# Writing the zero rows in eight pieces in steps 4 to 6, with batch 0's scatter moved to step 7

## What is computed

```python
p_packed = sm_attn(p, k, v)              # 8 batches, 8 heads: 32 packs attend to 576 tokens
out      = sm_attn(q, p_packed, p_packed)  # 576 tokens attend to the 32 packed values
x = out.transpose(0, 2, 1, 3).reshape(4608, 512)
# mixture of experts, the best one of 8 for each token
expert = argmax(x @ w_gate, axis=1)
x[expert == e] = gate * (relu(x[expert == e] @ w1[e]) @ w2[e])
# dense part on all tokens
r = relu(x @ w_in)                       # 512 -> 2048
y = (s * r * r + b) @ w_out              # 2048 -> 512
```

## Time and profile before

| | us |
|---|---|
| Median of three runs | 1540.14 |
| Lowest and highest | 1539.99 and 1545.33 |
| The profiled execution | 1553.64 |
| Its span, first to last instruction | 1551.9 |
| PE busy in the span | 1458.8 |
| Attention, to the last scatter issued | 197 |
| First slot's rows landed | 203.5 |

### The profile page before, as it was taken

One profiled execution on the slowest core, in us unless ns is written; L12 is line 12 of the kernel. 1 busy time (PEld: TensorE's weight loads), 2 busy tenths in 40 slices (PEclk: granted clock), 3 DMA queues, 4 the chain that ended last, 5 costly groups with the idle time before them and its releaser, 6 DMA issues.

```text
span 1551.9 us, 24717 instructions
## 1 busy us (share of the span) xinstructions
PE 1458.8 (94%) x8664; PEld 1174.5 (76%) x8665; DVE 474.2 (31%) x808; ACT 480.3 (31%) x973; POOL 415.6 (27%) x278
## 2 busy tenths in 40 slices
PE   6887369999999999998999999999999999999996
PEld 5655258888888888886888888888888888888885
DVE  3777621111111111113523232322323232332322
ACT  5666123333333333332222222222222222222221
POOL 0244678448266557104501010100101010010100
PEclk9899679999999999999999999999999999999998
DMA  9688345234243343212101010100101000000000
GB/s 309 220 264 250 120 147 159 87 108 133 70 141 108 109 122 115 81 48 90 61 14 42 7 41 14 38 10 14 41 8 41 14 34 14 14 27 0 27 1 27
DMA packets 52860, 122.93 MB, mean 79 GB/s; under 512 B 6609, under 2 KB 12753, under 8 KB 52817
## 3 DMA queue, kind: packets, MB, share of 16 engines
q1 hardware_dynamic: 33728, 79.21, 16.8%
q10 hardware_dynamic: 13136, 24.19, 5.1%
q0 software_dynamic: 5952, 18.92, 3.4%
HBM read 90.78 MB, written 31.52 MB: 79 GB/s over the span
## 4 chain that ended last, share of the span: by engine, by line
PE 90%; DVE 3%; issue 3%; DMA 1%; POOL 1%; ACT 1%; another core or an unknown queue 0%; SPq 0%; ACTq 0%; DVEq 0%; POOLq 0%
PE psum L674 18%; PE psum L676 18%; PE psum L675 18%; PE psum L750 8%; PE psum L748 8%; PE psum L749 8%; PE psum L718 2%; PE psum L507 1%; PE psum L683 1%; PE psum L736 1%; PE psum L568 1%; PE psum L547 1%; POOL x_by_expert L418 1%; PE psum L609 1%; PE psum L622 1%
## 5 line engine op out<-in xcount | busy, mean ns | idle before, releaser
L1241 DVE SCALAR_TENSOR_TENSOR s_r_r<-r_relu,s_col 128x512 f32<-128x512 f32 x144 | 116.1, 806 | 450.4 <-ACT r_relu L972 450.4
L482 POOL DMA_INDIRECT out_dram<-out_sb,out_row_of_y x36 | 36.0, 1001 | 747.2 <-ACT out_sb L982 739.0
L674 PE MATMUL psum<-weights_split,gT_hi 128*128 128x512 f32 x576 | 230.8, 401 | 2.3 <-DVE gT_lo L1243 2.2
L972 ACT ACTIVATE r_relu<-psum 128x512 f32<-128x512 f32 x144 | 86.1, 598 | 471.7 <-PE psum L750 456.9
L675 PE MATMUL psum<-weights_split,gT_hi 128*128 128x512 f32 x576 | 227.7, 395 | 0.0
L676 PE MATMUL psum<-weights_split,gT_lo 128*128 128x512 f32 x576 | 227.6, 395 | 0.0
L750 PE MATMUL psum<-yT_hi,weights_split 128*128 128x512 f32 x576 | 227.2, 394 | 0.0
L748 PE MATMUL psum<-yT_hi,weights_split 128*128 128x512 f32 x576 | 226.1, 393 | 0.1
L749 PE MATMUL psum<-yT_lo,weights_split 128*128 128x512 f32 x576 | 225.8, 392 | 0.0
L396 POOL TENSOR_TENSOR weights_split<-weights_raw,one 128x1024 fp32r<-128x1024 f32 x70 | 135.5, 1936 | 253.9 <-PE psum L676 242.7
L398 POOL TENSOR_TENSOR weights_split<-weights_raw,weights_split 128x1024 fp32r<-128x1024 f32 x70 | 170.0, 2428 | 5.5
(11 more groups left out here) (151 smaller groups left out, 1832.4 us busy)
## 6 DMA issues: line engine op xcount, KB each, us to landing
weights_raw<-in_moe_w_dram SPq DMA_DIRECT2D x64, 512.0 KB
x_slot<-x_by_expert ACTq DMA_DIRECT2D x40, 257.0 KB, 2.8
y_sorted<-y_slot ACTq DMA_DIRECT2D x40, 256.5 KB, 3.3
k_sb<-in_k_dram SPq DMA_DIRECT2D x16, 576.0 KB, 6.5
q_sb<-in_q_dram SPq DMA_DIRECT2D x16, 576.0 KB, 7.7
v_sb<-in_v_dram SPq DMA_DIRECT2D x48, 192.0 KB
y_tile<-y_sorted SPq DMA_DIRECT2D x32, 256.5 KB, 2.7
weights_raw<-in_moe_w_in_dram SPq DMA_DIRECT2D x8, 512.0 KB
```

Source lines behind the costliest of these rows:

```text
L674: nc.tensor.matmul(dst, lhs[0][:, col:col + P], rhs[0], start=first_, stop=False)
L972: nc.scalar.activation(rel[:], ps[:, HFB + par, :], ACT.Relu).then_inc(rel_done, 1)
L1241: nc.vector.scalar_tensor_tensor(sq[par][:], rel[:], s_col[:], rel[:], ALU.mult, ALU.mult).then_inc(sq_done, 1)
```

## The change

The single DMA of zeros ahead of step 0 is gone. ACT issues eight DMAs of 128 rows (257 KB) in its place: three in step 4, three in step 5, two in step 6, each group after `out_q` (and `exp_logits`) and before `out_pkt`. Each raises `zeroed` by 16, and POOL waits for 128. POOL no longer issues batch 0's scatters between the work of batches 1 and 2. It does `round_low(2)` after the sum of batch 1's logits, then the sum of batch 2's logits, the wait on `zeroed`, and all six scatters of batch 0 in a row, followed by batch 1's as before.

```diff
             for b in range(1, B):
                 u = 2 * b + 2
-                if b >= 2:
+                if b >= 3:
                     if b + 1 < B:
                         pool.wait_ge(pk_done, u + 1)
                     scatter(b - 2, 4)
...
                 sum_logits(b)
                 if b == 1:
-                    pool.wait_ge(zeroed, 16)
-                if b + 1 < B:
+                    round_low(2)
+                if b == 2:
+                    pool.wait_ge(zeroed, 16 * E)
+                    for j in range(J):
+                        scatter(0, j)
+                if 2 <= b and b + 1 < B:
                     scatter(b - 1, 0)
                     pool.wait_ge(m1_done, min(u + 3, UNITS))
                     scatter(b - 1, 1)
...
             out_kq(0)
-            act.wait_ge(zeros_done, 1)
-            act.dma_start(rows_dram.rearrange("(e r) c -> r e c", e=E)[0:P],
-                          zeros[:].unsqueeze(1).to_broadcast([P, E, XW])).then_inc(zeroed, 16)
             for it in range(UNITS + 1):
                 if it < UNITS:
                     out_q(it)
                 if it >= 5 and it % 2 == 1:
                     exp_logits((it - 5) // 2)
+                if it == 4:
+                    act.wait_ge(zeros_done, 1)
+                if 4 <= it < 7:
+                    for e in range(3 * it - 12, min(3 * it - 9, E)):
+                        act.dma_start(rows_dram[e * REG:e * REG + P, :], zeros[:]).then_inc(zeroed, 16)
                 if it >= 1:
                     out_pkt(it - 1)
```

## The result

| | kernel before | changed kernel |
|---|---|---|
| Median, 20 runs each (us) | 1543.38 | 1547.37 |
| Lowest and highest | 1538.49, 1547.04 | 1542.72, 1553.59 |
| Profiled execution | 1553.64 (see below) | 1547.03, span 1545.3 |

The ratio is 1.0028, with a 95% interval of 1.0016 to 1.0041: 4.0 us slower, where the prediction said 3.2 us faster. 1547.37 lies outside the range of 1533.5 to 1541.5; 3.2 us of the miss come from the base, since twenty runs of the kernel before have a median 3.2 us above the three first shown. The change stays within 0.5% of no change.

What follows compares the result with a forecast made beforehand. PE was taken to bound the kernel, with only the attention's end movable. Terms -3.7 + 0.5 + 0 + 0 = -3.2 us, from the median 1540.14, gave 1536.9, rounded to 1537 us; range 1533.5 to 1541.5.

Steps and rivals of the forecast that it cites:

- The gain of 3.7 us: Step 2: without the zeros, unit 3's keys come in time, saving 2.25 us idle and 1.48 us slow work.
- the 0.5 us for the pieces: ACT's issues in steps 4 to 6 delay the pack copy: 0.4, 0.1 and 0 us; bounds 0 and 1.1.
- the 0 for the gap in PE's loop: Step 4, gap at 52.78: an instruction fetch of fixed latency, so it stays 2.7 us; cost 0, between -2.7 and +2.4.
- the 0 for POOL: Step 8's scatter row: POOL's 2.4 us lag is made up and extra bytes make no keys late; cost 0.
- the experts and the dense part: Stages after the attention: they start when it ends and last as long as before, no change.
- Rival E: Step 2: unit 3's keys stay late behind q1's loads; only the 0.5 us of issues remains, 1540.6; chance 0.07.
- rival B: Steps 4 and 5: instruction page waits behind zeros in both, slow work after each; 7.8 us, 1544.7; chance 0.05.
- Rival C: The burst of scatters makes unit 10's keys late: +3.3 us, 1540.2; chance 0.07.
- the steps in question have no reason to differ: The median lies 13.5 us below the profiled span's execution; the changed steps were taken as equal in both.

Runs made afterwards that it cites:

- after: The changed kernel itself, with eight zero pieces and the new POOL order, against the kernel before: median 1547.37 us, ratio 1.0028; profiled execution 1547.03 us.
- dup_full: Kernel before plus six extra indirect stores of 96 rows of 514 floats on POOL in step 8, into a scratch tensor: ratio 1.0063.
- dup_tiny: Kernel before plus six extra indirect stores of 96 rows of only 8 floats on POOL in step 8, into a scratch tensor: ratio 1.0076.
- pool_only_3: Kernel before with only POOL's new order, six stores of batch 0 directly ahead of two of batch 1; zeros stay in front: ratio 1.0011.
- zeros_only_3: Kernel before with only the zeros changed to eight pieces on ACT in steps 4 to 6; POOL's order as before: ratio 1.0026.

## Why the prediction was wrong, point by point

The gain of 3.7 us had the right mechanism. What failed is the other side of the sum: the 0.5 us for the pieces, the 0 for the gap in PE's loop, the 0 for POOL, and the sentence that the experts and the dense part last as long as before.

**The zeros leave the first steps: right.** Step 2 went from 11.37 to 7.45 us, 3.9 us against a forecast of 3.7, with no wait for the keys and a full clock. Rival E is excluded by the same rows. In other traces with the zeros in front the lost time stands in step 1 or 2 and is up to 7 us, in four of them with no late keys (above).

**The pieces on ACT: the right mechanism, mis-sized.** The term was 0.5 us, from three issues of 0.46. They took 2.10, and PE's wait grew by 1.24 us (0.40 to 1.64) in step 4, where the sum had 0.4. The row of 0.46 was taken at 11.54, with the DMA engines as full as they ever were; in step 4 the first issue of the three took 1.01, for a reason that is not shown, and the bound of 1.1 rested on the same row.

**The gap at 52.78: the step chosen (fixed latency, 0) failed, and rival B's places were right with a smaller price.** In `after` the gap is 1.09 us longer (3.78 against 2.69), and a second of 1.46 came in step 5. Taken over all traces the first is less clear: 2.14 to 3.52 in the eleven traces with the zeros in front, 1.98 to 3.79 in the six with eight pieces on ACT, 4.80 and 3.53 with the 2.1 MB in one, 3.27 by SP. The second gap, of 0.79 to 2.00 us, is in five of those six and in one of the eleven (`dup_full`, 2.68). Steps 4 and 5 together went from 22.20 to 24.88, so that issues, gaps and slow clock made 2.7 us; the forecast had 0.5, rival B 7.8. Against the four traces of the lower level with the zeros in front (20.60 to 21.95) it is 3 to 4 us. That the instructions are what PE lacks is still read from the packet of the earlier trace rows, not shown.

**POOL: costed for its own lag and its bytes, and neither was the cost.** The lag of 2.4 us was indeed made up without anyone waiting for `round_low(3)`, and `dup_tiny` says that bytes don't matter. Not in the prediction were the standstill of the other engines beside the row (upper level, 8 to 9.5 us in step 8, 0.39% in all) and the meeting of L389 with DVE's addition (lower level, 2.36 us of DVE and 2.2 us of step 9).

**Late keys: right in kind, wrong in place and cause.** Rival C expected unit 10's keys to be late by the four more stores. They were not; unit 13's were, 2.49 us and a step of 12.67, as in three other traces of the lower level, of which one leaves the stores where they were and two the zeros, so that the change need not be what made them late. Here the sentence failed that "the steps in question have no reason to differ" between the profiled execution and the median of the runs: 13.5 us between the two were a warning that the trace came from another balance of the same kernel, and I subtracted them as a constant.

**The experts and the dense part: "last as long as before" failed.** 1351.40 us against 1348.35, of which 1.1 to 1.5 go with the eight DMA instructions on ACT, by the medians of seven traces against thirteen; the rest is inside what single traces scatter.

**The sum, as far as it can be made.** Both traces of the kernel before are of the other level; for the lower one `pool_only_3` and `zeros_only_3` come nearest. Between them the zeros won 5.0 us in steps 0 to 3 (here by the slow step 1 and the gap in step 2 of `pool_only_3`, not by late keys) and lost 4.0 in steps 4 and 5 and 2.5 from the first slot on; the rest, in steps 6 to 15, is 1.4 us the other way. With 1.5 us for the seam between the stages and the 2.2 of step 9, -5.0 + 4.0 + 1.5 + 2.2 = 2.7; measured were 4.0, with an interval of 2.5 to 6.3 (0.16 to 0.41%). Single executions differ by more than that in where their late load falls, and I don't settle the remainder. The step that was right is worth 4 to 5 us, and the places that were costed at 0.5 or left out eat more than all of it.

## What to carry to other kernels

Before a trace is used to price an edit, compare its time with the runs it stands for: 13 us too many meant that the odd steps had slack which the runs that count don't have. Work that is moved out of a stretch where it is seen to delay something has to be priced where it lands: the same issue that took 0.46 us ahead of step 0 took 1.09 and 2.42 in step 4, beside the one gap of PE that was there already. And fewer instructions are safer than smaller ones: one DMA of 2.1 MB on ACT cost 0.3% less than eight pieces of it, and six indirect stores moved to stand directly ahead of two others cost 0.4% on the upper level.

## What the runs showed of the hardware that I had not expected

- Indirect stores of 96 rows issued by POOL in a row, each 0.92 us, hold PE, ACT and DVE on two of the four chips of the experiments: 8 to 9.5 us in a step with eight, some 2.4 us in a step with three. Size doesn't matter (8 or 514 floats a row), and plain DMAs on POOL, 0.52 us each, do nothing of it. On the lower level the same program shows none of it (step 8 of 8.41 and 8.49 us).
- The issue of one DMA on ACT lasted 0.45 us for 4 KB and 0.46 for 2.1 MB ahead of step 0; in step 4 it was 0.97 to 2.19 for the first piece of 257 KB (0.34 to 0.59 for the seven after it) and 1.09 and 2.42 for the 2.1 MB. The share of the DMA engines did not tell which (1.03 beside the 0.46, 0.29 to 0.47 beside a 1.01).
- A DVE addition of 96 x 6 numbers took 2.52 us instead of 0.16 beside a POOL tensor operation of 2.36.
- Seven more DMA instructions in ACT's program moved another of its instructions by 0.30 us at a place 640 us later, always by the same; in six of seven traces a stretch of PE at half clock followed, worth 1.5 us, against three of thirteen without them.
